# The start of windowed attention in an attention and mixture-of-experts kernel: raw buffers, a queue, tables, a split and 46 matmuls

## The reference, cut to what matters

```python
scores = scale * np.matmul(q, k.transpose(0, 1, 3, 2))     # batch 2, heads 8, seq 768, head_dim 64
keep = is_global | is_local                                # first 8 keys, or the last 96 before the query
bias = -slopes[:, None, None] * dist[None, :, :]
scores = np.where(keep, scores + bias, -1e9)
a = softmax(scores);  attn = a @ v
x = attn.transpose(0, 2, 1, 3).reshape(1536, 512)
x = moe_dense(x)     # gates normalised 8 times over rows and columns, all 8 experts on all rows
out = moe_top1(x)    # each expert takes its 192 best tokens
```

## Time and profile before

| | us |
|---|---|
| three timed runs | 1589.9, 1597.81, 1608.67 |
| median | 1597.81 |
| the profiled execution's own time | 1607.92 |
| its span | 1606.2 |

### The profile page before, as it was taken

The page is one execution under the profiler, slowest core; times in us unless marked ns, Lnnn a source line. Parts: engine busy times, 40 slices in busy tenths (PEclk is TensorE's granted clock), DMA queues, the critical chain, the costliest instruction groups (busy, mean ns, idle before and its releaser), DMA issues.

```text
span 1606.2 us, 19153 instructions
## 1 busy us (share of the span) xinstructions
PE 1444.8 (90%) x7294; PEld 1200.4 (75%) x7294; DVE 652.0 (41%) x1574; ACT 344.0 (21%) x522; POOL 190.7 (12%) x177
## 2 busy tenths in 40 slices
PE   4999799999999999999999999999999333389998
PEld 3878588888888888888888888888887222278886
DVE  3353462332323323323233232332333788746663
ACT  2464322020121211102202112121111100034442
POOL 3241320010110101101001011010110200021210
PEclk9995899999999999999999999999999555589999
DMA  8451110110101101011011010110101300036660
GB/s 223 94 123 34 55 53 1 53 52 0 52 0 52 52 0 52 10 43 52 0 52 52 0 52 0 52 52 0 52 9 44 131 0 0 0 123 209 221 213 20
DMA packets 80021, 91.74 MB, mean 57 GB/s; under 512 B 36976, under 2 KB 43120, under 8 KB 79984
## 3 DMA queue, kind: packets, MB, share of 16 engines
q1 hardware_dynamic: 77936, 84.98, 16.7%
q0 software_dynamic: 2048, 6.29, 1.2%
HBM read 84.97 MB, written 6.29 MB: 57 GB/s over the span
## 4 chain that ended last, share of the span: by engine, by line
PE 87%; DVE 7%; issue 3%; DMA 1%; ACT 1%; POOL 1%; SPq 0%; DVEq 0%; ACTq 0%; POOLq 0%
PE PS L1202 25%; PE PS L1204 25%; PE PS L1203 25%; PE PS L1169 3%; PE PS L1294 2%; PE PS L1150 2%; PE PS L1140 2%; DVE G L965 1%; DMA kp<-in_kT 1%; PE PS L1216 0%; DVE xlo L825 0%; PE PS L1083 0%; DVE thr L963 0%; DVE lo L976 0%; PE PS L1317 0%
## 5 line engine op out<-in xcount | busy, mean ns | idle before, releaser
L1202 PE MATMUL PS<-xhi,w1hi 128*128 128x512 f32 (+1 forms) x1024 | 371.3, 363 | 3.4 <-DVE hlo L831 2.0
L1204 PE MATMUL PS<-xhi,w1lo 128*128 128x512 f32 (+1 forms) x1024 | 370.1, 361 | 0.0
L1203 PE MATMUL PS<-xlo,w1hi 128*128 128x512 f32 (+1 forms) x1024 | 370.0, 361 | 0.0
L1202 PE MATMUL PS<-w2hi,hhi 128*128 128x512 f32 (+1 forms) x896 | 349.5, 390 | 0.0
L1204 PE MATMUL PS<-w2hi,hlo 128*128 128x512 f32 (+1 forms) x896 | 349.3, 390 | 0.0
L1203 PE MATMUL PS<-w2lo,hhi 128*128 128x512 f32 (+1 forms) x896 | 349.0, 390 | 0.0
L591 ACT ACTIVATE hhi<-PS 128x512 fp32r<-128x512 f32 (+1 forms) x256 | 135.6, 531 | 901.6 <-PE PS L1204 901.6
L831 DVE SCALAR_TENSOR_TENSOR hlo<-PS,hhi 128x512 fp32r<-128x512 f32 (+1 forms) x256 | 155.6, 608 | 410.4 <-ACT hhi L591 410.0
L844 DVE SCALAR_TENSOR_TENSOR acc<-PS,prob_e,acc 128x512 f32<-128x512 f32 x192 | 144.0, 751 | 350.7 <-PE PS L1204 350.7
L1202 PEld LDWEIGHTS PS<-xhi,w1hi 128*128 128x128 f32 x1024 | 194.3, 190 | 37.3 <-DVE hlo L831 3.5
L1203 PEld LDWEIGHTS PS<-xlo,w1hi 128*128 128x128 f32 x1024 | 194.4, 190 | 30.4
(11 more groups left out here) (187 smaller groups left out, 933.1 us busy)
## 6 DMA issues: line engine op xcount, KB each, us to landing
raw<-in_w SPq DMA_DIRECT2D x64, 1024.0 KB, 5.4
qs<-in_qT SPq DMA_DIRECT2D x8, 384.0 KB, 4.1
kp<-in_kT SPq DMA_DIRECT2D x8, 384.0 KB, 5.0
vs<-in_v SPq DMA_DIRECT2D x16, 192.0 KB, 3.1
x_rows<-acc SPq DMA_DIRECT2D x3, 1024.0 KB, 12.0
kp<-in_kT SPq DMA_DIRECT2D x8, 240.0 KB, 4.9
vw<-in_v SPq DMA_DIRECT2D x16, 120.0 KB, 3.0
kp<-in_kT SPq DMA_DIRECT2D x8, 80.0 KB, 4.9
```

Source lines behind the costliest of these rows:

```text
L1202: T.matmul(o, whi, xh, start=first, stop=False)
L1203: T.matmul(o, whi, xl, start=False, stop=False)
L1204: return T.matmul(o, wlo, xh, start=False, stop=last)
```

## The change

1. Queries and keys have two raw buffers. Odd heads use the space of `raw2`, which is otherwise the raw buffer of the second expert weights. `load_qk(1)` is issued straight behind `load_qk(0)`, and `load_qk(h)` waits for the low parts of head h - 2 instead of head h - 1. The first two loads of second expert weights wait until all heads are split.
2. Values of head 0 are issued by ScalarE instead of SyncE, when GpSimd's first 15 constants are there.
3. The window tables take 14 steps instead of 17.
4. VectorE makes `klo` of head 0. GpSimd still makes its `qlo`.
5. TensorE runs 46 matmuls of constants (bf16, 512 columns) into a PSUM bank that is not yet in use, ahead of the read that chooses the path.

The diff, cut to its core:

```diff
+        raw2_flat = raw2[:].rearrange("p s k n -> p (s k n)")
+        q_raw = [qs[:], raw2_flat[:, 0:S]]
+        kp_flat = [kp[:].rearrange("p t c -> p (t c)"), raw2_flat[:, S:S + 2 * QT * P]]
...
+        ONES_SET = H + 7
...
             load_qk(0)
-            sp.wait_ge(s_const, H + 14)
-            load_v(0, 0)
-            load_v(1, 1)
-            sp.wait_ge(s_ql, 2)
             load_qk(1)
+            sp.wait_ge(s_const, ONES_SET)
+            load_v(sp, 1, 1)
             sp.dma_start(gate_raw[:, 0], ...)
             sp.dma_start(gate_raw[:, 1], ...)
-            load_w(0, 0, 0, 0)
-            load_w(0, 1, 1, 1)
             for h in range(2, H):
 
-                sp.wait_ge(s_ql, 2 * h)
+                sp.wait_ge(s_ql, 2 * h - 2)
                 load_qk(h)
+                if h == 3:
+                    load_w1(0, 0, 0, 0)
+                    load_w1(0, 1, 1, 1)
                 sp.wait_ge(s_ev, 2 * h - 1)
-                load_v(h, h % 2)
+                load_v(sp, h, h % 2)
+            sp.wait_ge(s_ql, 2 * H)
+            load_w2(0, 0, 0, 0)
+            load_w2(0, 1, 1, 1)
...
             for h in range(H):
                 pool.wait_ge(s_qh, 2 * h + 1)
-                pool.tensor_tensor(qlo[:, h % 2], qs[:], qhi[:, h % 2].bitcast(F32), ALU.subtract).then_inc(s_ql, 1)
-                pool.wait_ge(s_qh, 2 * h + 2)
-                pool.tensor_tensor(own_pages(klo, h % 2), kp_flat[:, P:], ...)
+                pool.tensor_tensor(qlo[:, h % 2], q_raw[h % 2], qhi[:, h % 2].bitcast(F32), ALU.subtract).then_inc(s_ql, 1)
+                if h:
+                    pool.wait_ge(s_qh, 2 * h + 2)
+                    pool.tensor_tensor(own_pages(klo, h % 2), kp_flat[h % 2][:, P:], ...)
...
+            act.wait_ge(s_const, ONES_SET)
+            load_v(act, 0, 0)
             act.wait_ge(s_const, H + 14)
 
             act.activation(negmax[:, 0:1], ident[:, 0:1], ACT.Exp).then_inc(s_tab, 1)
...
-                for j in range(2):
-                    own = slice(j * P, (j + 1) * P)
-                    dstep(V.tensor_tensor(pages[j], off[:, own], glob[:, 0:P], ALU.mult))
-                    dstep(V.tensor_tensor(pages[j], pages[j], rel[:, own], ALU.add))
+                dstep(V.tensor_tensor(pages[:, 0:2], off, far.unsqueeze(1).to_broadcast([P, 2, P]), ALU.mult))
+                dstep(V.tensor_tensor(pages[:, 0:2], pages[:, 0:2], rel, ALU.add))
...
-                dve.wait_ge(s_qk, 16 * QK_LOADS * (h + 1))
+                dve.wait_ge(s_qk[h % 2], 16 * QK_LOADS * (h // 2 + 1))
...
+                if h == 0:
+                    dve.wait_ge(s_qh, 2)
+                    V.tensor_tensor(own_pages(klo, 0), kp_flat[0][:, P:], own_pages(khi, 0).bitcast(F32), ALU.subtract
+                                    ).then_inc(s_ql, 1)
...
+            def spin(n, width=4 * P):
+
+                for _ in range(n):
+                    T.matmul(PS[:, 7, 0:width].rearrange("p (a b) -> p a b", b=P), tri[:],
+                             tri[:].unsqueeze(1).to_broadcast([P, width // P, P]), start=True, stop=True)
...
+            spin(46)
             path(pe, lambda is_narrow: attend_window() if is_narrow else attend_full())
```

More of the change, by code:

```diff
@@ L310, in own_keys, with load_v @@
             return x[rows, par, 3 * c:3 * c + 3, P:2 * P]
+        ONES_SET = H + 7
+        def load_v(eng, h, par):
+            vb = v[h].rearrange("(t p) (b d) -> p t b d", p=P, b=B)
+            for b in range(B):
+                eng.dma_start(vs[:, par, :, b, 0:D], vb[:, :, b]).then_inc(s_vl[par], 16)
+                eng.dma_start(vw[GK:P, par, :, b, 0:D], vb[GK:P, 0:QT - 1, b]).then_inc(s_vl[par], 16)
+                eng.dma_start(vw[0:GK, par, :, b, 0:D], vb[0:GK, 0:1, b].to_broadcast([GK, QT - 1, D])
+                              ).then_inc(s_vl[par], 16)
         w1_v = w1.rearrange("e (c p) f -> e p c f", p=P)
@@ L322, in load_qk @@
                 kb = kT[h].rearrange("d (t c) -> d t c", c=P)
[L323 to L334, removed]
@@ L336, in load_w @@
-            def load_w(e, half, par, u):
+                q_in, k_in = q_raw[h % 2], k_raw[h % 2]
+                sp.dma_start(q_in, qT[h]).then_inc(s_qk[h % 2], 16)
+                sp.dma_start(k_in[:, :, P:2 * P], kb).then_inc(s_qk[h % 2], 16)
+                sp.dma_start(k_in[:, 1:QT, GK:P], kb[:, 0:QT - 1, GK:P]).then_inc(s_qk[h % 2], 16)
+                sp.dma_start(k_in[:, 1:QT, 0:GK], kb[:, 0:1, 0:GK].to_broadcast([B * D, QT - 1, GK])
+                             ).then_inc(s_qk[h % 2], 16)
@@ L696, in window_tables @@
             def window_tables():
-                global_distances(slice(0, P))
-                rel, loc, off = dt1[:, 0:2 * P], dt1[:, 2 * P:4 * P], dt2[:, 0:2 * P]
-                pages = [dist[:, 0, j * P:(j + 1) * P] for j in range(5)]
+                m[0] = N_COMMON
+                pages = dist[:, 0, 0:5 * P].rearrange("p (j c) -> p j c", c=P)
+                rel, loc, off = (x.rearrange("p (j c) -> p j c", c=P) for x in (dt1[:, 0:2 * P], dt1[:, 2 * P:4 * P], dt2[:, 0:2 * P]))
+                far = glob[:, 0:P]
+                dstep(V.tensor_scalar(far, colk[:, 0:P], lim[:, 1:2], MASKED, ALU.is_ge, ALU.mult))
+                dstep(V.tensor_scalar(far, far, lim[:, 0:1], None, ALU.max))
                 for j in range(2):
-                    dstep(V.tensor_scalar(dt1[:, j * P:(j + 1) * P], colk[:, 0:P], -1.0, rowq[:, j:j + 1], ALU.mult, ALU.add))
+                    dstep(V.tensor_scalar(rel[:, j], colk[:, 0:P], -1.0, rowq[:, j:j + 1], ALU.mult, ALU.add))
                 dstep(V.tensor_scalar(loc, rel, 0.0, None, ALU.is_ge))
```

37 lines of the change are left out of this document (21 added, 16 removed).

## The result

| | before | after |
|---|---|---|
| executions | 20 | 20 |
| median of all, us | 1606.24 | 1588.43 |
| lowest and highest, us | 1589.14, 1634.91 | 1578.47, 1620.54 |
| ratio of the compared executions | | 0.9921, 95% interval 0.9891 to 0.9950 |

By this ratio the change makes the kernel faster by 0.8%. The ratio, here and in the table of the experiments, compares only the faster executions of each kernel, so where the times scatter it says nothing of the median; the medians of all differ by 17.8 us, or 1.1%. Ten of the 20 executions after lie between 1585.9 and 1589.8, within 3.9 us; of those before at most five lie as close together.

The account below looks back on a forecast made before the run. TensorE was taken as the bound, with 105 of attention's 143 us at the lower clock level. From 1607.9 us, 22 for the first three heads and 5.5 for the second low stretch gave 1580; range 1564 to 1606.

Parts of the forecast that it names:

- case 1: Attention: higher clock level held over the start, lost once later; 1580 us, between 1572 and 1588; chance 0.38, the forecast.
- Case 3: Before the first scores: level lost in the idle hole, scores begin low; 1604 or 1594 us; chance 0.37.
- The 7.5: Attention heads: a head of six steps costs 7.5 us more at the lower clock level.
- case 2: Attention: higher level held throughout, another 18 us for the second low stretch; 1568 us; chance 0.16.
- Case 4: Slower: level lost in the hole and back later than 77 us; 1619 or 1627 us; chance 0.09.
- Start of VectorE: Kernel start: six DMA issues ahead of ScalarE's table load delay VectorE by 2.5 us, bounds 1.5 to 4.5.
- Tables: Window tables before the first scores: three fewer steps, two of the rest twice as wide; 0.8 us saved.
- Split: Head 0's subtractions: VectorE and GpSimd exclude one another, so splitting them saves 1.35 us and not 3.1.
- Second raw buffer: Head 1: its keys land before VectorE asks, so the stall of 3.7 to 4.1 us goes.
- the waits of steps 19 and 31: Later heads: VectorE's waits for keys stay, since `load_qk(h)` still stands behind `load_v(h - 1)`.
- The 46 matmuls' own time: TensorE before the scores: start at 4.35, end at 16.7 us, or 24.3 if the level never rose.
- What lies behind 184 us: After attention: nothing behind 184 us changes its length.

Follow-up runs that it names:

- E2: The changed kernel with 74 leading constant matmuls in place of 46; median 1587.4 us.
- E4: E3 with 52 leading matmuls in place of 46; median 1580.1 us.
- E3: The changed kernel with ScalarE's table load and exponential ahead of its six issues of head 0's values; median 1575.9 us.
- E10: E3 with the next head's queries and keys issued ahead of the head's values; median 1581.3 us.
- E5: E4 with 7 constant matmuls ahead of head 0's first value matmuls; median 1577.7 us.
- E6: E4 with 15 constant matmuls in four places of steps 0 to 2; median 1585.5 us.
- E7: E6 with SyncE issuing the next head's queries and keys ahead of the head's values; median 1563.0 us.
- E1: The changed kernel without its 46 matmuls; median 1602.7 us.
- B1: The kernel before with the 46 matmuls only; median 1591.0 us.
- E11: The changed kernel with 15 constant matmuls in the pipeline's filling and the next head's keys issued ahead of values; median 1572.2 us.
- E8: E7 without its 52 leading matmuls, the 15 in the filling kept; median 1566.1 us.
- E14: E8 with head 0's second subtraction (`klo`) back on GpSimd; median 1568.4 us.
- E12: The changed kernel with 15 constant matmuls in the pipeline's filling, loads in the change's order; median 1582.3 us.
- before again: The kernel before, unchanged, profiled a second time; 1590.7 us.
- E9: The changed kernel with only the next head's queries and keys issued ahead of the head's values; median 1592.9 us.
- E13: E8 without its 15 constant matmuls, so with none at all; median 1583.2 us.

## Why the prediction was wrong

**The failed step: the choice of case 1.** It put the first three heads at the higher level because the 46 matmuls raise it and a hole of 3.5 us might be survived, and drew 22 us from that. Case 3 ("Lost in the hole") is what happened to the level: the first three heads take 13.6, 20.1 and 20.4 us. Two things were wrong with the choice. The hole is 6.41 us, since the term before it was mis-sized (below). And it would have failed with a small hole as well: E2 and E4 have none before the scores, E3 and E10 small ones of 0.75 and 1.47 that they survive, and all four lose the level at the next gap of 1.46 or 1.47 us, in the filling of the pipeline, which the working never looked at. E5, E6 and E7, with that gap filled, keep it. In the trace of before it lies inside the stall at 29.10, and shows only when the stall is gone and the level high: the change, at the lower level, has 0.31 us there, E2 and E4 have 1.47.

**The size of case 3.** "What is left is the stall less the later start: 3.5" gives 1604, or 1594 with the median's stretches; measured is 1588.4. The level at the first scores was taken for all that the matmuls are worth. E1 shows that they move the median by 14 us (4 to 20) though the level is lost before the scores, and B1 points the same way, less surely. What they shift, as far as the profiles and the mean clocks tell, is when it comes back and whether it stays. The groups are 8 to 10 us apart. The 7.5 set head 2 at the lower level (20.5) against heads 3 and 4 at the higher (13.0), which do more. Heads 1 and 2 take 11.55 and 12.00 in E11 and 20.10 and 20.44 in the change, so there a head costs 8.5, which is within the groups' distance. The term that the profiled pair shows, the second low stretch, was priced right (18 us; measured 19.7 from head 3 on), but was given to case 2 alone.

That 1588.4 lies inside the range of 1564 to 1606, and next to case 1's own, is luck: case 1's mechanism did not come, and case 3's time was undercut by a course of the level that no case had.

**Case 4**, the other side, did not come in the median. Two of the change's 20 executions (1612.3 and 1620.5) are of its size.

**Start of VectorE: +2.5, bounds 1.5 to 4.5; measured +5.07, outside.** The six issues took 6.6 us. ScalarE's and SyncE's sequencers, in the changed kernel:

```profile
3.95 1.34 ACTq L322 DMA_DIRECT2D vw<-in_v  x1
5.31 0.68 ACTq L320 DMA_DIRECT2D vs<-in_v  x1
6.02 2.22 ACTq L321 DMA_DIRECT2D vw<-in_v  x1
8.27 1.18 ACTq L322 DMA_DIRECT2D vw<-in_v  x1
...
4.14 2.76 SPq L337 DMA_DIRECT2D raw<-in_qT  x1
6.95 0.56 SPq L338 DMA_DIRECT2D raw<-in_kT  x1
7.54 1.56 SPq L339 DMA_DIRECT2D raw<-in_kT  x1
9.15 1.57 SPq L340 DMA_DIRECT2D raw<-in_kT  x1
```

SyncE's last four issues before 18.8 us take 0.44 to 0.54 each; here they take up to 2.76. I chose a value near the end at which nothing holds them, and the nearer row was the held one. The rule of the Trainium skill that the prediction weighed ("Perfetto Trace Analysis", section "DMA Instruction — HWDGE (DVE, Sync)": an issue locks the descriptor generator for itself) gave 4.6, and was nearer. That the two engines alternate, as I had read it, the trace doesn't bear out. In E8 four of ScalarE's issues pass while one of SyncE's stands:

```profile
4.32 0.44 ACTq L320 DMA_DIRECT2D vs<-in_v  x1
4.79 0.87 ACTq L321 DMA_DIRECT2D vw<-in_v  x1
5.69 0.52 ACTq L322 DMA_DIRECT2D vw<-in_v  x1
6.23 0.55 ACTq L320 DMA_DIRECT2D vs<-in_v  x1
...
4.15 2.63 SPq L337 DMA_DIRECT2D raw<-in_qT  x1
...
9.35 3.79 SPq L320 DMA_DIRECT2D vs<-in_v  x1
```

SyncE's issue at 9.35 takes longest of all, most of it after ScalarE's last has ended at 10.20. Three of SyncE's issues in turn (6.82 to 9.31) pass while one of ScalarE's stands at 6.81 (2.79 us). What holds them is open; it was there in the kernel before, with SyncE alone (2.48).

The cost of this step is more than its 5 us. E3, where the exponential goes ahead, has its first scores 5.1 us sooner and is 12.6 us below the change (resampled, 5 to 21).

**Tables: -0.8; measured -0.78** (13.00 to 17.97 against 5.75). Right.

**Split: -1.35; measured -1.6**, in the change and in E14. The exclusion was right in the main: `klo` takes 3.10 us, where it would take 1.71 alone, and ends 1.5 us behind the end of `qlo`. From the end of the `khi` cast the two take 3.13 us (19.34 to 22.47), where the working had 3.4 or more, and 1.7 without exclusion. The Trainium skill's page "SBUF — State Buffer", section "Terms", says that VectorE and GpSimd share a port pair that one of them holds for a whole instruction; the trace agrees with that but for 0.3 us.

The three terms sum to the measured shift of the first scores: 5.07 - 0.78 - 1.61 = 2.68.

**Second raw buffer: -3.7 to -4.1; measured -3.9** on head 0. Right. For later heads I expected the waits of steps 19 and 31 to stay. In the profiled execution, where the heads before were slow enough for the loads, step 19 has none, step 25 has 0.31 us and step 31 has 0.39. Where the level is high early the waits are back, in step 13 already, at 2.2 to 2.9 us (E5, E6, E12), by the cause that the working gave, `load_qk` behind `load_v`. The buffer pays in full only with E7's order.

**The 46 matmuls' own time: end 16.7; measured 16.11.** Right. **What lies behind 184 us** should not have changed; it grew by 2.5 us, with a gap of 3.17 before the second group of expert matmuls where before has 1.98. Behind the longer one the granted clock is at 0.50 from 175.0 to 178.4, which before does not show. That gap is 0.81 to 3.17 in the profiles of this study, of kernels with the same program there, so I do not put it down to the change.

**What stays open:** why the leading matmuls, whose level is lost in the hole, make the return at the end of head 2 without a later loss more frequent (ten of 20 executions in the one group) than it is without them. One profile each of before, B1, before again and the change have the return at 76 to 78; E2, E4 and E10 have it at the end of head 2 as well, at 69 to 74; E1, E3 and E9, of which two have the matmuls, have it at 95 to 108. I have no run that ties the two together, and ten profiles are too few for frequencies. It matters less than it seems: with constant matmuls at the right place and the keys in time (E8, E11) no execution came back late.

## What to carry to other kernels

Matmuls that lift the clock are worth most where no gap follows them: follow TensorE through the whole filling of the pipeline, and put constant matmuls into the gaps there rather than ahead of a wait; then look for the load that becomes late at the higher level, since here neither step paid clearly without the other. Price DMA issues on a second engine by the rows where issues are held, and put nothing that others wait for behind them. Where times come in groups, find the groups and what separates them before giving an edit a price, since a median moves by the share of the groups. The mean granted clock of each execution can tell them apart where one profile cannot, as far as the low stretches print.

## What the runs showed of the hardware

- 15 constant matmuls of some 0.2 to 0.4 us each in the first three steps were worth 16 us and took the scatter from 42 us to 2 (the change against E11, with the order of the loads).
- The length of a gap alone did not decide whether the level was lost. In attention it was lost behind gaps of 0.89 (before again, at 111.4), 1.27 (E1), 1.32 (before), 1.46 or 1.47 (E2, E3, E4, E10), 1.74 (E5), 2.17 (E6), 2.41 (E12) and 6.41 us (the change), and kept over one of 1.28 (E6, at 77.8) and, behind dense 512-column matmuls, over one of 1.47 (E10, at 16.0).
- Behind the dense first group of expert matmuls it took more. In the 18 profiles the level was kept over the eleven gaps of 0.81 to 2.38 us (before has 1.98) and lost behind the seven of 2.48 to 3.17 (E11 has 2.48):

```profile
194.66 0.50 PE L1202 MATMUL PS<-xhi,w1hi 128*128 128x512 f32 x1 [1.98 <-DVE hlo L831]
158.05 0.50 PE L1239 MATMUL PS<-xhi,w1hi 128*128 128x512 f32 x1 [2.48 <-DVE hlo L858]
```

- The fall can come some time behind the gap: 2.4 us behind its end in E10, 2.7 in before again, 0.2 in E4.
- At the lower level it can stay down 48 us without any gap (the change, 28 to 76 us), and it can come back behind a few matmuls of the same program (E13, at 22.8).
